# Attention scan and two expert layers on one core: keys loaded ahead of receptances, the first quarter of w_in subtracted on GpSimd, VectorE's order in the prologue and the first masks one turn sooner

## What is computed

```python
# r, k, v, w: (4, 8, 768, 48); u: (8, 48)
for t in range(S):
    cur = einsum('bhd,bhe->bhde', u[None] * kt, vt)
    y[:, :, t] = einsum('bhd,bhde->bhe', rt, state + cur)
    state = wt[:, :, :, None] * state + einsum('bhd,bhe->bhde', kt, vt)
x = y as (3072, 384)
h = x @ w_in                                  # (384, 2048)
x = (maximum(h, 0) + alpha * minimum(h, 0)) @ w_out   # (2048, 384)
e = argmax(x @ w_gate, 1); p = softmax(x @ w_gate)[e]  # 8 experts
out = p * (maximum(x @ w1[e], 0) @ w2[e])     # (384, 1024), (1024, 384)
```

## Time and profile before

| | |
|---|---|
| median of 3 runs | 787.7 us |
| lowest, highest | 787.44, 795.22 us |
| the profiled execution | 791.64 us |
| its span, first to last instruction | 789.8 us |
| its mean granted TensorE clock | 0.979 |
| busy: PE, PEld | 737.8 us (93%), 518.4 us (66%) |
| busy: DVE, ACT, POOL | 469.9 us (59%), 364.5 us (46%), 391.7 us (50%) |
| transferred | 171.61 MB, mean 217 GB/s |
| chain that ended last | PE 66%, DMA 8%, DVE 7%, POOL 5%, issue 5%, ACT 3% |

### The profile page before, as it was taken

One profiled execution on the slowest core, in us unless ns is written; L12 is line 12 of the kernel. 1 busy time (PEld: TensorE's weight loads), 2 busy tenths in 40 slices (PEclk: granted clock), 3 DMA queues, 4 the chain that ended last, 5 costly groups with the idle time before them and its releaser, 6 DMA issues.

```text
span 789.8 us, 17773 instructions
## 1 busy us (share of the span) xinstructions
PE 737.8 (93%) x6779; PEld 518.4 (66%) x6779; DVE 469.9 (59%) x959; ACT 364.5 (46%) x734; POOL 391.7 (50%) x372
## 2 busy tenths in 40 slices
PE   4689989989999989999989999997999999999995
PEld 3447655656765666665666666656787878878783
DVE  7995877677768777786786763464433333333331
ACT  3652576647646756646756664462121221212210
POOL 6452567769759759778768875352010101101011
PEclk9987999999999999999999999998999999999998
DMA  8838318372653653645545245797799776776763
GB/s 345 330 131 236 134 62 298 110 250 92 220 213 119 231 211 121 230 140 193 193 151 180 80 160 191 285 419 271 259 394 381 282 246 223 239 263 214 251 232 115
DMA packets 42838, 171.61 MB, mean 217 GB/s; under 512 B 5214, under 2 KB 13152, under 8 KB 37120
## 3 DMA queue, kind: packets, MB, share of 16 engines
q1 hardware_dynamic: 30160, 108.18, 38.8%
q10 hardware_dynamic: 9072, 52.09, 18.7%
q0 software_dynamic: 3520, 10.17, 3.3%
HBM read 133.87 MB, written 37.33 MB: 217 GB/s over the span
## 4 chain that ended last, share of the span: by engine, by line
PE 66%; DMA 8%; DVE 7%; POOL 5%; issue 5%; ACT 3%; SPq 1%; ACTq 1%; POOLq 0%; DVEq 0%
PE bank L1687 5%; PE bank L1689 5%; PE bank L1688 5%; PE bank L1675 5%; PE bank L1676 5%; PE bank L1678 5%; PE bank L1833 4%; PE bank L1831 4%; PE bank L1832 4%; PE bank L1796 4%; PE bank L1797 4%; PE bank L1798 4%; DMA arena<-w_exp_dram 4%; PE bank L1647 2%; DMA route_rows<-xrow,pos 2%
## 5 line engine op out<-in xcount | busy, mean ns | idle before, releaser
L594 POOL TENSOR_TENSOR act_buf<-act_buf 128x384 f16<-128x384 f32 x128 | 119.6, 934 | 148.7 <-ACT act_buf L793 147.8
L1267 DVE SCALAR_TENSOR_TENSOR act_buf<-neg,slope,bank 128x384 f32<-128x384 f32 x128 | 77.8, 608 | 89.4 <-ACT neg L786 88.9
L1687 PE MATMUL bank<-arena,act_buf 128*128 128x392 f16 x384 | 128.2, 334 | 1.5 <-POOL act_buf L594 1.0
L682 POOL DMA_INDIRECT out_dram<-neg,dest x28 | 27.6, 984 | 203.0 <-DVE neg L1520 195.4
L1689 PE MATMUL bank<-arena,act_buf 128*128 128x392 f16 x384 | 128.1, 334 | 0.0
L1688 PE MATMUL bank<-arena,act_buf 128*128 128x392 f16 x384 | 128.1, 334 | 0.0
L1675 PE MATMUL bank<-xh,arena 128*128 128x384 f16 x384 | 126.8, 331 | 1.3 <-DVE act_buf L1267 0.6
L1676 PE MATMUL bank<-xl,arena 128*128 128x384 f16 x384 | 126.7, 331 | 0.0
L1796 PE MATMUL bank<-shared,arena 128*128 128x128 f16 x672 | 116.5, 221 | 1.4 <-DMA arena<-expert_split 1.4
L1797 PE MATMUL bank<-shared,arena 128*128 128x128 f16 x672 | 116.5, 221 | 0.0
L1798 PE MATMUL bank<-shared,arena 128*128 128x128 f16 x672 | 116.4, 221 | 0.0
(11 more groups left out here) (174 smaller groups left out, 1552.3 us busy)
## 6 DMA issues: line engine op xcount, KB each, us to landing
arena<-expert_split ACTq DMA_DIRECT2D x29, 1536.0 KB, 8.2
...
```

Of the source, the lines that this page charges most:

```text
L594: pool.tensor_tensor(gl[:, f % 4, :], gf[:, f % 4, :], gh[:, f % 4, :], ALU.subtract).then_inc(gl_done, 1)
L1687: pe.matmul(at, gh[:, f % 4, ts], woh[:, f, :], start=(f == 0), stop=False)
```

## The change

- **Transfers.** Keys and receptances of the first two chunks, one transfer of 512 KB each before, are two of 256 KB; the keys go ahead (`load_first_k`), with semaphores of their own. GpSimd's `decayed_k` waits for keys alone and `decayed_q` for receptances. The first half of w_out is loaded ahead of the tokens of chunk 2 instead of two transfers later. The first expert transfer waits for `w_in_lo0` too.
- **First quarter of w_in.** `first_w_in_high` on ScalarE scales the quarter in place, makes its high part, and then the second quarter's, three instructions of 1536 columns instead of one of 3072. `first_w_in_low` on GpSimd subtracts, 1536 columns, in place of `w_in_low(0, 0)` on VectorE. `hidden(0)` waits for it.
- **Order of VectorE in the prologue.** The first masks stand ahead of the scan of chunk 2, the inverses of chunk 2 behind `v_low(0, 0, 0)`, `row_sums` one place or more sooner, `w_out_low(0, 0)` ahead of the next half's first scan, the next half's first inverses and second scan in turns 0 and 3.
- **First turns.** GpSimd scales the next half's first keys in turn 0 behind `hidden_low`. TensorE makes `outputs(0)` ahead of the scores. Masks and both `att_low` of chunk 0 stand in turn 2 instead of 3 and 4; `low_k` and `turned_k` in turn 3; `w_in_high(1)` in turn 3 instead of 1. For chunks 1 and 2 of that half the second `att_low` stands in the turn of the masks.

The diff, its small semaphore lines cut:

```diff
@@ -354,8 +358,13 @@
...
                     sp.sem_inc(sp_went, 1)
-                src = rk_in[m] if isinstance(b, int) else rk_in[bass.ds(m, 1)].rearrange("o d k n -> (o d) k n")
-                sp.dma_start(rk_sb[:, (half + c) % 2, :, :], src).then_inc(rk_arrived[(half + c) % 2], 16)
+                if m < 2:
+                    sp.dma_start(rk_sb[:, m, 0, :], rk_in[m][:, 0, :]).then_inc(rk_arrived[m], 16)
+                else:
+                    sp.dma_start(rk_sb[:, m % 2, :, :], rk_in[m]).then_inc(rk_arrived[m % 2], 16)
+            def load_first_k(m):
+                sp.dma_start(rk_sb[:, m, 1, :], rk_in[m][:, 1, :]).then_inc(first_k_in[m], 16)
@@ -395,8 +404,10 @@
...
             load_w(0, 0, 0, True)
+            load_first_k(0)
...
             load_rk(0, 0, 0, True)
+            load_first_k(1)
@@ -407,9 +418,9 @@
...
             load_v(0, 0, 2, True)
+            sp.dma_start(wide[3], w_out[0]).then_inc(wide_in[3], 16)
...
             load_w(0, 1, 0)
-            sp.dma_start(wide[3], w_out[0]).then_inc(wide_in[3], 16)
@@ -539,13 +551,19 @@
...
                 pool.wait_ge(inv_done, m + 1)
-                pool.wait_ge(rk_arrived[at], 16 * (3 * b + (3 * half + c) // 2 + 1))
+                if m < 2:
+                    pool.wait_ge(first_k_in[m], 16)
+                else:
+                    pool.wait_ge(rk_arrived[at], 16 * (m // 2 + 1))
...
             def decayed_q(b, half, c):
+                m = 6 * b + 3 * half + c
+                if m < 2:
+                    pool.wait_ge(rk_arrived[m], 16)
@@ -587,6 +605,12 @@
...
                                    ).then_inc(unit_lo, 1)
+            def first_w_in_low():
+                fs = slice(0, FF // 4)
+                pool.wait_ge(w_in_hi0, 1)
+                pool.tensor_tensor(first_w_in(0, wil)[:, :, fs], wide[0].rearrange("p (k n) -> p k n", k=KD)[:, :, fs],
+                                   first_w_in(0, wih)[:, :, fs], ALU.subtract).then_inc(w_in_lo0, 1)
@@ -607,8 +631,7 @@
...
                 diagonal(0, 0, c)
-            decayed_k(0, 1, 0)
-            decayed_q(0, 1, 0)
+            first_w_in_low()
@@ -623,6 +646,9 @@
...
                         if start:
+                            if f == 0:
+                                decayed_k(nb, nh, 0)
+                                decayed_q(nb, nh, 0)
@@ -769,6 +795,16 @@
...
                 act.activation(gcol[0:NE, q * 512:(q + 1) * 512], b_gc[0:NE, :], ACT.Copy).then_inc(gc_copied, 1)
+            def first_w_in_high():
+                part = lambda i: (slice(None), slice(None), slice(i * FF // 4, (i + 1) * FF // 4))
+                src = wide[0].rearrange("p (k n) -> p k n", k=KD)
+                act.wait_ge(wide_in[0], 16)
+                act.activation(src[part(0)], src[part(0)], ACT.Copy, scale=WIS).then_inc(w_in_scaled, 1)
+                act.wait_ge(w_in_scaled, 1)
+                act.activation(first_w_in(0, wih)[part(0)], src[part(0)], ACT.Copy).then_inc(w_in_hi0, 1)
+                act.activation(first_w_in(0, wih)[part(1)], src[part(1)], ACT.Copy, scale=WIS).then_inc(hi_done, 1)
@@ -857,7 +893,7 @@
...
             gate_cols_copy(0)
-            w_in_high(0)
+            first_w_in_high()
@@ -883,20 +919,24 @@
...
                             exps(g - 1)
-                        if start and f == 0:
+                        if start and f == 1:
                             decayed_keys(0, 1, 0)
-                        if start and f == 1:
-                            w_in_high(1)
...
                                 decayed_keys(nb, nh, 1)
-                            if f % 4 == 3 and f < 15:
+                            if f % 4 == 3 and f < 15 and not (start and f == 3):
...
                                 att_high(nb, nh, c, 1, b_y)
-                            if f % 4 == 0 and f > 0 and update(nh, c):
+                            if start and f == 2:
+                                att_high(nb, nh, 0, 0, b_s)
+                                att_high(nb, nh, 0, 1, b_y)
+                            if f % 4 == 0 and f > 0 and update(nh, c) and not (start and f == 4):
                                 turned_k(nb, nh, c, b_s)
+                            if start and f == 3:
+                                turned_k(nb, nh, 0, b_s)
+                                w_in_high(1)
@@ -1271,26 +1311,37 @@
...
                         if start and f == 0:
-                            w_out_low(0, 0)
+                            gate_cols_low(0, b_gt[:, 0:8 * NE])
+                            inverses(0, 1, 0)
...
                             inverses(nb, nh, 2)
-                        if f == 2:
+                        c = (f - 3) // 4
+                        if start and f == 2:
+                            mask(nb, nh, 0, 0, b_s)
+                            mask(nb, nh, 0, 1, b_y)
+                            att_low(nb, nh, 0, 0, b_s)
+                            att_low(nb, nh, 0, 1, b_y)
+                        if f == (3 if start else 2):
                             v_low(nb, nh, 0)
-                        c = (f - 3) // 4
-                        if f % 4 == 3 and f < 15:
+                        if f % 4 == 3 and f < 15 and not (start and f == 3):
...
                             att_low(nb, nh, c, 0, b_s)
+                            if start:
+                                att_low(nb, nh, c, 1, b_y)
                         if start and f == 3:
+                            low_k(nb, nh, 0, b_s)
+                            decays(0, 1, 1, b_hid[f][:, 0:C])
...
                         if f % 4 == 0 and f > 0:
-                            att_low(nb, nh, c, 1, b_y)
-                            if update(nh, c):
+                            if not start:
+                                att_low(nb, nh, c, 1, b_y)
+                            if update(nh, c) and not (start and f == 4):
@@ -1402,14 +1453,14 @@
...
             inverses(0, 0, 1)
-            decays(0, 0, 2, bank[4][:, 0:C])
...
             mask(0, 0, 0, 1, b_y)
-            inverses(0, 0, 2)
+            decays(0, 0, 2, bank[4][:, 0:C])
...
             v_low(0, 0, 0)
+            inverses(0, 0, 2)
@@ -1420,29 +1471,26 @@
...
             v_low(0, 0, 1)
+            row_sums(0, 0, 1)
...
             mask(0, 0, 2, 1, b_y)
-            row_sums(0, 0, 1)
...
             state(0, 0, 1, b_o[1])
+            row_sums(0, 0, 2)
...
             v_low(0, 0, 2)
-            row_sums(0, 0, 2)
             decayed_state(0, 0, 2)
-            w_in_low(0, 0)
+            dve.wait_ge(alpha_in, 16)
+            dve.tensor_scalar(slope[:, :], alpha_sb[:, :], -1.0, 1.0, ALU.mult, ALU.add).then_inc(slope_done, 1)
...
             low_x(0, 0, 2, b_o[2])
+            w_out_low(0, 0)
             decays(0, 1, 0, b_y[:, 0:C])
-            inverses(0, 1, 0)
-            decays(0, 1, 1, b_y[:, 0:C])
-            gate_cols_low(0, b_gt[:, 0:8 * NE])
-            dve.wait_ge(alpha_in, 16)
-            dve.tensor_scalar(slope[:, :], alpha_sb[:, :], -1.0, 1.0, ALU.mult, ALU.add).then_inc(slope_done, 1)
@@ -1707,6 +1757,9 @@
...
                             hidden(nb, nh, f + 3 - NF, False, last and half == 0, last)
+                        if start and f == 0:
+                            pe.wait_ge(w_out_ready, 2)
+                            outputs(g, f)
@@ -1717,7 +1770,7 @@
...
                                     if c == 0 and start:
-                                        pe.wait_ge(scan_done, NC + 2)
+                                        pe.wait_ge(scan_done, NC + 1)
@@ -1738,12 +1791,13 @@
...
                             turn(f // 15)
-                        if start and f in (0, 4):
-                            pe.wait_ge(w_out_ready, 2 + f // 4)
+                        if start and f == 4:
+                            pe.wait_ge(w_out_ready, 3)
                         if start and f in (8, 12):
-                            pe.wait_ge(wide_free[0], 1 + f // 4)
+                            pe.wait_ge(wide_free[0], f // 4)
                             pe.wait_ge(w_out_ready, 4)
-                        outputs(g, f)
+                        if not (start and f == 0):
+                            outputs(g, f)
@@ -1769,7 +1823,7 @@
...
             gate_cols(1, 2)
-            pe.wait_ge(wide_free[0], 1)
+            pe.wait_ge(w_in_lo0, 1)
```

11 lines of the change are left out of this document (9 added, 2 removed).

## The result

The changed kernel is slower by 0.8%: 796.38 us median of 20 runs against 789.59 for the kernel before, also 20 runs on the same chip, ratio 1.0079, 95% interval 1.0059 to 1.0098, or +6.2 us (+4.7 to +7.7). The forecast was +2.0, or 789.7 us, in a range of 784 to 796. The median itself came out 0.4 us above the range's end; the ratio times the 787.7 from which the forecast was made gives 793.9, inside it. The narrower range of the forecast's own mechanism, 787 to 793 at 0.50, was missed by both. "Within 1%", at 0.88, came true. So the time lies in the wide range only, with three times the forecast change.

A forecast was written before the change was run, and what follows sets the result against it. TensorE was taken as the steady-state bound, with VectorE releasing nearly all its waits in the prologue and first turns. Terms 3.5 + 0.6 + 2.0 - 2.0 - 1.5 - 0.6 = +2.0 on 787.7 gave 789.7 us, range 784 to 796.

The forecast's parts named there:

- the forecast's own mechanism: Whole kernel: the summed terms hold as told, time 787 to 793 us, chance 0.50.
- Within 1%: Whole kernel: time changes by no more than one per cent, 7.9 us, either way, chance 0.88.
- Prologue, +3.5 forecast: Prologue: first hidden matmul starts near 43.4 us instead of 39.96, +3.5 us.
- the hold of v_low: Prologue, chunk 2: GpSimd's subtract holds VectorE's v_low until 38.15, so the attention starts +3.5 us instead of +1.7.
- the first rival: Prologue: GpSimd's subtract comes after v_low(2) or does not hold it; prologue costs 1.7, time 785.8 us, chance 0.22.
- +1.7, for VectorE's order and ScalarE's three passes: Prologue: attention of chunk 2 at 36.3 for 34.65 without the hold, ScalarE's passes ending at 32.8; +1.7 us.
- Part 1, keys first: 0: Start of prologue: sooner keys gain nothing, since first scores start where the warm-up matmuls end; 0, bounds -0.3 and +0.5.
- Part 6, w_out loaded ahead of tok of chunk 2: 0: Prologue loads: later tokens cost nothing, being first used after 30 us and covered by chunk 1's products; 0, bounds 0 and +1.
- masks before 14: Start of prologue: first masks before 14 us, where 15.0 was expected, was a sign that the forecast is wrong.
- Rival B: Prologue: clock falls behind TensorE's idling, scores and transposes at half clock add about 3, time 792.7 us, chance 0.20.
- Part 4: Turns 0 to 5: late_gate_cols waits for y_rows and starts at 70.4, +0.6 us; lower clock behind it, +2.0.
- Part 5: Turns 6 to 12: waits for att_low go in turn 10 (-2.0) and turn 6 (-0.6), low clock behind turn 10 (-1.5).

The follow-up runs named there:

- e7: Changed kernel with row_sums of chunks 1 and 2 and the w_out/token load order as before, GpSimd's subtract kept; ratio 1.0046 against before.
- e3: Changed kernel with w_in's first quarter made on VectorE again, one ScalarE pass for three, no GpSimd subtract in the prologue; ratio 1.0046 against before.
- e1: Changed kernel's loads, prologue and GpSimd subtract kept, turns 0 to 15 of the first half in the old order; ratio 1.0053 against before, +4.2 us.
- e2: Kernel before with only turns 0 to 15 of the first half changed, old loads and prologue; ratio 1.0006, +0.5 us.
- e10: Kernel before with one edit, both att_low of a chunk in one turn in the first half; ratio 0.9989, -0.9 us.
- e12: Kernel before with both att_low in one turn and VectorE's casts of constants moved from turn 13 to turn 6; ratio 0.9970, -2.4 us.
- e5: Kernel before, unchanged, run again for a second profile; ratio 1.0008.
- e8: Kernel before with only its first loads changed, keys and receptances of chunks 0 and 1 in two transfers, keys ahead; ratio 1.0008.
- e9: Changed kernel with 44 extra warm-up matmuls filling TensorE's idle time in the prologue; ratio 1.0098 against before, over 7 runs.
- e11: Changed kernel with the outputs matmuls of turn 3 moved ahead of late_gate_cols; ratio 1.0062 against before.

## Why the prediction was right or wrong

**Prologue, +3.5 forecast.** One of its two parts was right, the hold of v_low: w_in_hi0 was there at 29.3, long before 35.8, so the first rival did not come; the subtract takes 3.10 (3.1 forecast), v_low well over 2 us (2.08), and hidden comes at 43.22 (43.4). The other part, +1.7 for VectorE's order and ScalarE's three passes, was not: the passes take 1.47, 1.49 and 1.47 us (4.25 in all forecast) but end at 30.7, not 32.8, and e7, which keeps them, has the attention of chunk 2 at 34.27. What held att_low(2), at 32.04, was row_sums(2) (31.46 + 0.55); in e7 it starts at 31.19. The Trainium skill's rule in "SBUF — State Buffer", "Who interferes with whom", by which the first of the two engines keeps the port pair to its end, is borne out here by e3, 0.55 against 2.08. The cost is 5.0 us over the profiles and +4.2 in time (e1). That 43.22 came so near 43.4 is partly luck. Two steps stand behind it:
- *The base.* 39.96 came from one execution in which u_rep landed at 9.24. In the other five profiles with the old prologue the first hidden comes 1.3 us sooner in the mean. "Part 1, keys first: 0" rested on the same profile, with the first scores right at the end of the warm-up. That holds in e2, e10 and e12 too; in e5 and e8 GpSimd's products hold the scores (1.61 and 0.30 us). The value 0 was right (e8), its reason holds in some executions and not in others.
- *Part 6, w_out loaded ahead of tok of chunk 2: 0.* The cover that I named, the products of chunk 1, ends at 25.5 while the tokens land at 29.34. The wait of 1.15 is handed to row_sums(2), which the change had put ahead of att_low(2). I had used row_sums(2) only as what lets the subtract go, and had asked nothing of its own input.

In the order of VectorE the parts were off and cancelled: first masks at 11.79 and not at 15.0, scores of chunk 2 at 22.69 and not at 24.6. By my own sign "masks before 14" the step was to be called wrong, and it was.

**Rival B, the clock falls in the prologue, 0.20.** It did fall, in every profile with the whole new prologue. Its price of 3 us isn't borne out: e9 moved the low clock to another place and gained nothing. What remains is that the changed kernel's mean clock over all runs is 0.004 to 0.005 lower, which at TensorE's full load would be 3 to 4 us of 790 by my estimate. Against that sum stands e9, whose mean clock of 0.980 is nearly that of before and whose time is +0.98%. Which stretches of it count at the end is open.

**Part 4, +0.6 and +2.0 for the clock.** late_gate_cols waited 2.92 for the forecast "over 4" and began 2.93 later than before instead of 4.1. Their length of 9.09 against 5.93 says that a clock cost of the forecast's kind is there, in this stretch. e11, which halves the wait, shortens that stretch by 1.5 us.

**Part 5, -4.1: the step that failed most.** The waits went as told: turn 10 from 2.00 to none, turn 6 from 0.94 to 0.72, clock 1.00 from 104 to 108. Alone it is worth 0.9 us, at most 2.8 (e10), and with the casts moved 2.4 (e12, -0.9 to -3.9); both exclude the -4.1. The sum treated TensorE's saved waiting as the kernel's gain, while VectorE and GpSimd set the pace right behind: row_sums of the next half waits for GpSimd, whether the casts ahead of it are held or not (0.36 and 3.79 us, e10 and e12), and the scan behind it 3 us for w in both profiles. I never followed the gain past turn 12. In e10's profile some 2.6 us of it reach the next half; what becomes of the rest in time stays open.

**The sum put right.** With e1 for the prologue and e10 for part 5 it is +2.0 + (4.2 - 3.5) + (4.1 - 0.9) = +5.9, for +6.2 measured. Both terms put in have intervals of 2 us to each side, and with e12's 2.4 in place of 0.9 it would be +4.4, so the close agreement is partly luck. Parts 4 and 5 together would have been -1.5 and are +0.5 (e2). What stays open is e7: hidden only 0.5 us later than the old prologue's mean, and still 3.6 us slower than before (1.5 to 5.8), 18 us of its profile at a clock of 0.53. Whether its other executions lose time there too isn't shown.
